# A new order of attention's work on all queues, and the first layer's first two tiles inside the last head

## What is computed

```python
# attention, B, H, S, D = 2, 8, 768, 64
q_bits = (q @ proj > 0); k_bits = (k @ proj > 0)       # 6 bits each -> bucket
mask = q_bucket[..., :, None] == k_bucket[..., None, :]
scores = where(mask, q @ k.T / sqrt(D), -1e9)
scores -= scores.max(-1)
attn = exp(scores); attn /= attn.sum(-1) + 1e-9
x = attn @ v                                           # -> [1536, 512]
# first layer, 512 -> 2048 -> 512
h = maximum(x @ w_in, 0.0); y = h * h @ w_out
# second layer: 8 experts, capacity 192 tokens each, assigned greedily by logit
out[tokens of e] = maximum(y[tokens of e] @ w1[e], 0.0) @ w2[e]
```

## Time and profile before

| | |
|---|---|
| median of 3 runs | 866.53 us (862.17 to 868.55) |
| the profiled execution | 864.65 us, its span 862.9 us, mean granted TensorE clock 0.951 |
| attention | from 0 to about 297 us |
| first layer | to about 582 us |
| routing and experts | to the end |
| busy over the span: DVE, ACT, POOL | 44%, 44%, 46% |

### The profile page before, as it was taken

One profiled execution on the slowest core, in us unless ns is written; L12 is line 12 of the kernel. 1 busy time (PEld: TensorE's weight loads), 2 busy tenths in 40 slices (PEclk: granted clock), 3 DMA queues, 4 the chain that ended last, 5 costly groups with the idle time before them and its releaser, 6 DMA issues. The chain is left out here.

```text
span 862.9 us, 14217 instructions
## 1 busy us (share of the span) xinstructions
PE 787.4 (91%) x4720; PEld 715.8 (83%) x4720; DVE 378.7 (44%) x875; ACT 378.3 (44%) x655; POOL 399.5 (46%) x326
## 2 busy tenths in 40 slices
PE   5999989879996979999999999995399999999986
PEld 3799878768885768999999999984399999899986
DVE  7465656545663245242232224224554455345500
ACT  2676757556674555554554554540012112212221
POOL 5578757565764768655565666560100110111001
PEclk8999999999998989999999999996589999999999
DMA  6465475483845000010000001000343635364531
GB/s 163 101 151 122 108 164 128 102 188 86 192 102 156 1 0 1 0 38 0 0 37 0 0 0 38 0 0 37 131 177 122 230 136 212 118 226 138 192 139 36
DMA packets 43687, 81.38 MB, mean 94 GB/s; under 512 B 17176, under 2 KB 17176, under 8 KB 43136
## 3 DMA queue, kind: packets, MB, share of 16 engines
q1 hardware_dynamic: 41440, 74.58, 30.8%
q0 software_dynamic: 2048, 6.29, 2.2%
q10 hardware_dynamic: 160, 0.00, 0.0%
HBM read 54.55 MB, written 6.29 MB: 71 GB/s over the span
## 5 line engine op out<-in xcount | busy, mean ns | idle before, releaser
L310 POOL TENSOR_TENSOR pt_lo<-pt,pt_hi 128x768 fp32r<-128x768 f32 x64 | 117.7, 1839 | 58.9 <-ACT pt_hi L438 56.5
L1122 PE MATMUL banks<-xt_hi,split_parts 128*128 128x384 f32 (+1 forms) x512 | 141.7, 338 | 0.0
L1133 PE MATMUL banks<-split_parts,h_hi 128*128 128x512 f32 x384 | 122.8, 401 | 5.3 <-DVE h_lo L1048 5.2
L886 POOL TENSOR_TENSOR split_parts<-w_in_sb,split_parts 128x512 fp32r<-128x512 f32 x64 | 84.4, 1319 | 90.3 <-ACT split_parts L879 89.0
L1045 DVE TENSOR_TENSOR h<-relu 128x384 f32<-128x384 f32 x64 | 43.5, 680 | 182.5 <-ACT relu L1000 182.5
L431 ACT ACTIVATE pt<-banks 128x768 f32<-128x768 f32 x96 | 78.0, 813 | 75.5 <-PE banks L683 74.3
L544 DVE TENSOR_REDUCE mx<-banks 128x1 f32<-128x768 f32 x96 | 90.5, 956 | 28.5 <-PE banks L710 24.4
L1566 PE MATMUL banks<-x_cols,w_in_sb 128*128 128x192 f32 x512 | 95.8, 339 | 1.2 <-ACT x_cols L1346 1.1
L1122 PEld LDWEIGHTS banks<-xt_hi,split_parts 128*128 128x128 f32 x512 | 93.7, 188 | 2.9
L1580 PE MATMUL banks<-expert_hidden,w_out_sb 128*128 128x192 f32 x512 | 94.6, 336 | 0.0
L890 POOL TENSOR_TENSOR split_parts<-w_out_sb,split_parts 128x512 fp32r<-128x512 f32 x64 | 84.2, 1315 | 16.2 <-ACT split_parts L882 16.2
(11 more groups left out here) (195 smaller groups left out, 1355.0 us busy)
## 6 DMA issues: line engine op xcount, KB each, us to landing
w_in_sb<-in_moe_w SPq DMA_DIRECT2D x8, 2048.0 KB, 9.8
w_out_sb<-in_moe_w SPq DMA_DIRECT2D x8, 2048.0 KB, 8.6
w_in_sb<-in_moe_w_in SPq DMA_DIRECT2D x8, 512.0 KB, 7.3
w_out_sb<-in_moe_w_out SPq DMA_DIRECT2D x8, 512.0 KB, 5.7
w_out_sb<-in_k SPq DMA_DIRECT2D x16, 192.0 KB, 4.1
w_out_sb<-in_q SPq DMA_DIRECT2D x16, 192.0 KB, 3.4
v_raw<-in_v SPq DMA_DIRECT2D x16, 192.0 KB, 3.8
ka<-split_parts SPq DMA_DIRECT2D x16, 192.0 KB, 4.0
```

The source lines that it names most:

```text
L310: pool.tensor_tensor(pt_lo[x % 2][:], pt[j % 2][:], pt_hi[x % 2][:].bitcast(fp32), ALU.subtract).then_inc(los, 1)
L886: pool.tensor_tensor(wil[i], in_view(f), wih[i].bitcast(fp32), ALU.subtract).then_inc(wils, 1)
L1122: last = pe.matmul(PB[i][:, 0:HALF], w_[:, k, :], x_[:, xs], start=n == 0, stop=n == 3 * DT - 1)
L1133: last = pe.matmul(PB[2 + t][:], h_[:, tc], w_[:], start=start and n == 0, stop=stop and n == 2, skip_group_check=True)
```

## The change

On SyncE the weight transfers go one to each call of `weights` (n from 2 to 13, before: 4 to 12 with two at n = 9 to 11), ka goes ahead of free_row and qb, and the loads of k and q stand behind ka and v. On ScalarE `k_high` stands ahead of the exponential of tile 1, `high(p - 1)` behind that of tile 5, and the first splits of w_in and w_out are in pair 6 and no longer in pair 7. GpSimd follows. TensorE and VectorE have some neighbours exchanged. `hidden` of steps 0 and 1 stands in the last head, with their relu and square between its exponentials; the last head's sums, copy to xt, divisors and low part stand behind the first layer's first steps.

```diff
@@ SyncE
             def weights(n):
-                if 4 <= n < 12:
-                    load_in(sp, n - 4)
-                if 9 <= n < 13:
-                    load_out(sp, n - 9)
+                if 2 <= n < 10:
+                    load_in(sp, n - 2)
+                elif 10 <= n < 14:
+                    load_out(sp, n - 10)
...
             for p in range(PAIRS):
+                asm_kb(2 * p + 1, 1)
+                part_ka(1, p % 2)
                 if p:
                     free_row(2 * p - 1, 1)
-                asm_kb(2 * p + 1, 1)
-                part_ka(1, p % 2)
                 asm_qb(2 * p + 1, 1)
                 if p:
                     load_v(2 * p + 1, 1)
+                weights(2 * p)
                 part_qa(1, p % 2)
+                weights(2 * p + 1)
                 if p + 1 < PAIRS:
                     asm_kb(2 * p + 2, 0)
                     asm_qb(2 * p + 2, 0)
                     free_row(2 * p, 0)
+                    part_ka(0, (p + 1) % 2)
+                    load_v(2 * p + 2, 0)
+                more_k(p + 3)
                 more_q(p + 3)
-                weights(2 * p)
-                if p + 1 < PAIRS:
-                    load_v(2 * p + 2, 0)
-                    part_ka(0, (p + 1) % 2)
-                more_k(p + 3)
-                weights(2 * p + 1)
                 if p + 1 < PAIRS:
                     part_qa(0, (p + 1) % 2)
@@ GpSimd
             for p in range(PAIRS):
-                if p:
-                    low(p - 1)
+                if p + 2 < PAIRS:
+                    k_low(pool, p + 2)
                 low_part(2 * p, 1)
...
                 v_low_part(2 * p + 1, 1)
                 if p + 2 < PAIRS:
                     q_low(pool, p + 2)
-                    k_low(pool, p + 2)
+                if p + 2 == PAIRS:
+                    split["in_low"](pool, 0, 0, 0)
+                    split["in_low"](pool, 1, 1, 1)
+                    split["out_low"](pool, 0, 0, 0)
+                if p:
+                    low(p - 1)
                 low_part(2 * p + 1, 1)
...
-                if p + 1 == PAIRS:
-                    split["in_low"](pool, 0, 0, 0)
-                    split["in_low"](pool, 1, 1, 1)
-                    split["out_low"](pool, 0, 0, 0)
                 divide(p, 0)
                 divide(p, 1)
...
-            low(PAIRS - 1)
+            later["low"] = lambda: low(PAIRS - 1)
@@ ScalarE
             for p in range(PAIRS):
                 expo(2 * p, 0)
-                high(p - 1)
                 sums(2 * p - 1, 1)
+                k_high(p + 2)
+                if p + 2 == PAIRS:
+
+                    for taken in (ka_in, kb_in, qa_in, qb_in):
+                        act.wait_ge(taken[0], 32 * (PAIRS - 1) - (16 if taken in (kb_in, qb_in) else 0))
+                        act.wait_ge(taken[1], 32 * (PAIRS - 1))
+                    act.wait_ge(split["w_early"], 16 * 9)
+                    split["in_high"](act, 0, 0)
+                    split["in_high"](act, 1, 1)
+                    split["out_high"](act, 0, 0)
                 expo(2 * p, 1)
                 expo_high(2 * p, 1)
-                k_high(p + 2)
...
                 expo(2 * p, 4)
-                if p + 1 == PAIRS:
...
+                v_high(2 * p + 1, 1)
                 expo_high(2 * p, 4)
                 expo(2 * p, 5)
+                high(p - 1)
+                row(2 * p + 1, 1)
                 q_high(p + 2)
-                row(2 * p + 1, 1)
                 v_sum_high(2 * p + 1)
-                v_high(2 * p + 1, 1)
...
                 expo(2 * p + 1, 4)
+                if p + 1 == PAIRS:
+                    split["tile"](act, 0, 0)
                 expo_high(2 * p + 1, 4)
                 expo(2 * p + 1, 5)
-                v_sum_high(2 * p + 2)
                 row(2 * p + 2, 0)
                 v_high(2 * p + 2, 0)
-            sums(HEADS - 1, 1)
-            high(PAIRS - 1)
+                v_sum_high(2 * p + 2)
+            split["tile"](act, 1, 1)
+            later["sums"] = lambda: sums(HEADS - 1, 1)
+            later["high"] = lambda: high(PAIRS - 1)
@@ VectorE
+                    q_bits(p + 1, qbit[w]).then_inc(qbits, 1)
                     k_bits(p + 1, kbit[w]).then_inc(kbits, 1)
-                    q_bits(p + 1, qbit[w]).then_inc(qbits, 1)
...
+                sum_v(2 * p + 1, 1)
                 row_max(2 * p + 1, 5)
-                sum_v(2 * p + 1, 1)
...
-            turn(HEADS - 1, 1, 0)
-            turn(HEADS - 1, 1, 1)
-            reciprocals(HIGH)
-            dve.drain()
+            def last_divisors(h):
+                turn(HEADS - 1, 1, h)
+                if h:
+                    reciprocals(HIGH)
@@ TensorE
+            def early_hidden(g):
+
+                if g == 0:
+                    pe.wait_ge(mxs, 6 * HEADS - 1)
+                    pe.wait_ge(xl, 5)
+                split["hidden"](pe, g, 0, g)
+
             def pair(p, w, first, last):
 
-                if not last:
-                    z_k(p + 1, w)
+                if not first:
+                    weigh(2 * p - 1, 1, 5)
                 scores_t(2 * p, 0, p, 0)
                 if not first:
-                    weigh_low(2 * p - 1, 1, 4)
-                    weigh(2 * p - 1, 1, 5, False, True)
-                scores_t(2 * p, 0, p, 1)
+                    weigh_low(2 * p - 1, 1, 4, False, True)
                 if not last:
                     z_q(p + 1, w)
+                    z_k(p + 1, w)
+                scores_t(2 * p, 0, p, 1)
                 weigh(2 * p, 0, 0, True)
...
                 weigh(2 * p, 0, 5)
+                weigh_low(2 * p, 0, 4)
                 scores_t(2 * p + 1, 1, p, 0)
-                weigh_low(2 * p, 0, 4)
                 weigh_high(2 * p, 0, 4, False, True)
...
                 scores_t(2 * p + 1, 1, p, 2)
+                if last:
+                    early_hidden(0)
...
+                fallback(2 * p + 1, 1, 0)
+                scores_t(2 * p + 1, 1, p, 4)
+                if last:
+                    early_hidden(1)
                 weigh_low(2 * p + 1, 1, 1)
-                scores_t(2 * p + 1, 1, p, 4)
-                fallback(2 * p + 1, 1, 0)
-                weigh_high(2 * p + 1, 1, 3)
                 weigh_low(2 * p + 1, 1, 2)
                 fallback(2 * p + 1, 1, 1)
+                weigh_high(2 * p + 1, 1, 3)
@@ weight_splits: hidden and tile, used by both stages
+    def tile(act, g, i):
+        act.wait_ge(hid, g + 1)
+        act.activation(r32[i][:], PB[i][:, 0:HALF], ACT.Relu).then_inc(relus, 1)
+        act.wait_ge(relus, g + 1)
+        act.activation(hh[i][:], r32[i][:], ACT.Square).then_inc(hhs, 1)
@@ first layer, GpSimd
             for g in range(6):
                 both_low(g, g + 2, g + 1, g % 2)
+                if g == 1:
+                    later["low"]()
@@ first layer, ScalarE
-                tile_high(c * FT, 2, 1, 0, None if first else c - 1)
-                tile_high(c * FT + 1, 3, 2, 1)
                 if first:
+
+                    in_high(2, 2, 0)
+                    out_high(1, 1, 1)
+                    later["sums"]()
+                    in_high(3, 3, 1)
+                    out_high(2, 2, 0)
+                    later["high"]()
                     for g in range(2, 8):
                         tile_high(g, g + 2, g + 1, g % 2)
@@ first layer, VectorE
                     if first:
-                        if j == 1:
+                        if j < 2:
+                            later["divisors"](j)
+                        elif j == 3:
@@ first layer, TensorE
-            hidden(0, 0, 0)
             chunk(0, 0, HALF, True, False)
```

More of the change, by code:

```diff
@@ L93, in attention @@
         more_bits = sb("more_bits", [P, S])
+        later = {}
         kbit = (spare[:, SPARE + 2 * S:SPARE + 3 * S], spare[:, SPARE - S:SPARE])
@@ L615, in pair @@
                     row_max(2 * p + 2, 5)
+                    sum_v(2 * p + 2, 0)
                     max_done(2 * p + 2)
-                    sum_v(2 * p + 2, 0)
                 invert(p)
@@ L639, in _ @@
             pair(PAIRS - 1, 0, False, True)
-            turn(HEADS - 1, 1, 0)
-            turn(HEADS - 1, 1, 1)
-            reciprocals(HIGH)
-            dve.drain()
+            def last_divisors(h):
+                turn(HEADS - 1, 1, h)
+                if h:
+                    reciprocals(HIGH)
+            later["divisors"] = last_divisors
         @block.tensor
@@ L837, in _ @@
             pair(PAIRS - 1, 0, False, True)
-            weigh_low(HEADS - 1, 1, 4)
-            weigh(HEADS - 1, 1, 5, False, True)
+            weigh(HEADS - 1, 1, 5)
+            weigh_low(HEADS - 1, 1, 4, False, True)
+        return later
 def routing_constants(nc, ctx):
@@ L870, in weight_splits, with hidden @@
     wihs, wils, wohs, wols = (sem("split_" + n) for n in ("wihs", "wils", "wohs", "wols"))
+    hid, relus, hhs = (sem("first_" + n) for n in ("hid", "relus", "hhs"))
```

(50 more changed lines are left out.)

41 lines of the change are left out of this document (17 added, 24 removed).

## The result

| | before | changed kernel |
|---|---|---|
| median | 865.95 us (862.17 to 868.55, 4 runs) | 837.34 us (835.10 to 841.54, 4 runs) |
| ratio | | 0.9679, 95% interval 0.9626 to 0.9731 |
| profiled execution | 864.65 us, span 862.9 | 841.54 us, span 839.8 |

The forecast was 837 (828 to 849).

What follows compares the result with a forecast made beforehand. TensorE, busy 91% of the span, was taken as the bound, so only its stalls could be won: 36.3 us removed less 6.7 back, net 29.6, from the 866.53 us median to 837 us (828 to 849).

Steps and rivals of the forecast that it cites:

- Part 1: Order of the loads on SyncE: TensorE's waits for qa in pairs 3 to 6 go, 19.2 us removed.
- Part 2: Copy to xt_hi behind the head's scores: the last pair's first half loses 9.5 us, with 0.4 us back.
- The wait that I named next: Last pair: first weigh waits for VectorE's two transposes with only four matmuls as cover, 0.4 us back.
- Part 3: k_high ahead of the exponential of tile 1 on ScalarE: fits between sums and tile 1's scores, priced at 0.
- Part 4: First weight splits moved to pair 6: ScalarE waits for qa, TensorE idles 4.6 us; cost 6.3 us, bounds 2 and 9.
- Part 5: Two first-layer tiles inside the last head: h_lo wait and half-clock rows(0) go, 7.1 us, plus 0.5 for pt_lo.
- rival C: Entry of the first layer keeps a wait, 3 to 5 us with half clock: 841 us, chance 0.10.
- the sign of being wrong on part 5: Entry of the first layer: h_lo or the low part of w_in is waited for.
- A: Pair 6's wait does not appear, as ScalarE's wait ends within TensorE's cover: 831 us, chance 0.16.
- D: Nothing is won, since the stalls come back elsewhere in the cycle: 858 to 866 us, chance 0.07.
- B: The load queue stays late and half of the 19.2 us remains: 847 us, chance 0.14.
- E: Pairs 0 to 5: ScalarE's wait for ka ahead of tile 1's exponential stalls TensorE; 871 us at 9 us landing, chance 0.03.

Runs made afterwards that it cites:

- The old order: The kernel with the late splits, with TensorE's and VectorE's order within a pair as before the change: 826.92 us, and 828.37 us when run again.
- the kernel with a gap of 3.85: The changed kernel with pair 6's two weight transfers behind all its other loads: 833.71 us.
- the late splits: The changed kernel with the first weight splits later, ScalarE's behind the odd head's row copy in pair 6, GpSimd's at pair 7's start: 829.48 and 828.47 us.

## Why the prediction was right

**Part 1** (19.2 us forecast). Right in mechanism and size: 18.5 us in pairs 1 to 5, 19.5 with the loads alone. The sum of bytes behind asm_kb against 247 GB/s was enough to see that qa would be in time. In pair 2 of the changed kernel its last half is issued at 107.20 us and lands 4.6 us later, 29.5 us into the pair, where I had 27 and TensorE wants it at 33.

**Part 2** (9.5 less 0.4). 8.6 us measured. The wait that I named next is there, but for the exponential of tile 1 and not for the transposes: 0.55 us at 251.63 in the changed kernel, with scores_t of that tile now right behind weigh_low. The old order shows the wait for the transposes instead, 0.6 us. Either way half a microsecond.

**Part 3** (0). Right. ScalarE shows no wait ahead of its copy of k in any pair of the changed kernel: in pair 1 it starts at 57.29 us, as the sums end.

**Part 4** (6.3 back, bounds 2 and 9). Right in mechanism, undersized: 10.1 us (26.85 less the 16.72 of a first half without a stall), just past my upper bound. Two terms were short. The landing: I took it at 235.0 us, 10.8 after the pair's start at 224.16, and it came 13.7 after (219.46 less 205.72), 2.9 late, by the two weight transfers beside qa and by scatter. And the half clock: I took 1.7 us from pairs 3 and 5. Here it was 2.7 (10.13 less 7.43) and, in the kernel with a gap of 3.85, 2.7 too (its first half took 23.24). Pairs 4 and 7 had shown more before: 5.59 of excess for 3.52 of idle, 9.53 for 6.79. I had these rows and took the cheaper ones.

**Part 5** (7.6 with the wait for pt_lo). 7.67 us: the size is right, and the wait for h_lo is gone as forecast. But I wrote the gain up as the tiles covered by their place, and that is 1.0 of it. The rest lies in what stood ahead of relu, GpSimd's three splits, the division, the sums and the copy. I had named that chain as the cause of the wait, but gave the splits' leaving it to part 4, as a cost alone; which link is worth how much stays open. A wait of 0.50 us for w_in's low part, behind GpSimd's divisions, is what I had as rival C, at a tenth to a sixth of its price; I had also set a wait for that low part as the sign of being wrong on part 5, and by it the part is not clean. VectorE's h steps in the last head were shorter than feared: 0.56 and 0.56 us for the first tile (GpSimd had nothing then), 0.56 and 1.49 for the second; the earlier trace rows had 1.75 for one beside GpSimd.

```profile
276.43 0.56 DVE L1089 TENSOR_TENSOR h<-relu 128x384 f32<-128x384 f32 x1 [7.30 <-ACT relu L908]
277.06 0.56 DVE L1092 TENSOR_TENSOR h_lo<-h,h_hi 128x384 fp32r<-128x384 f32 x1
...
283.79 1.49 DVE L1092 TENSOR_TENSOR h_lo<-h,h_hi 128x384 fp32r<-128x384 f32 x1
```

**The sum.** In the profiled executions I forecast -29.6 us. Up to the end of the first layer it was -26.3, 3.3 short, nearly all of it part 4; the second layer added 3.2 that have nothing to do with the change, -23.1 in all. The medians differ by 28.6. That 837 was met to 0.3 us is in part luck, then: part 4 cost 4 us more than I said in its profile, and the median ran lower than the profile by as much. Of the rivals, A and D did not happen, B and E left no trace, C happened at 0.5 us.

## What to carry to other kernels

Where an engine is full between its stalls, cut its time at a repeated event and price each stretch against the cleanest one: what an order can win is the excess. More than half of it was had here by moving transfers alone (19.5 of the 36 us that the late splits win up to there). A wait in an in-order queue costs by what stands behind it; here one block of 1.7 us of work, put one position too early behind a transfer, cost 10 us of TensorE, six times itself, and moved half a pair later it was free. When a large edit wins, take its parts singly: the loads, the copy, and what no longer stands ahead of the first relu carry nearly all of it, and the exchanged neighbours on TensorE and VectorE nothing. And take them apart to the end: what was won at the end of attention, 6.7 us of it, is left with two possible causes, because the move that looked like a pure cost (the weight splits, out of pair 7) may also be what freed GpSimd at the end of attention.

## What the runs showed of the hardware that was not expected

- The same code scatters in its transfers' landing: 6.9, 6.4 and 4.9 us for pair 6's qa (192 KB) in three profiles of the same code up to there, with a transfer of 512 KB ahead of it and one behind. Without them it took 3.8 and 4.3 us in two.
- The second layer, the same tensor work in all kernels here, took from 274.2 to 281.8 us from the first layer's last matmul on h_hi to the end, over 14 profiles. Single profiles of two kernels can differ by 7 us with no cause in the change. In the two profiles at the ends of this range TensorE's weight loads waited 3.3 and 6.8 us for the gathered rows, which is half of the difference; the other half stays open.
- What the half clock adds does not follow the length of the gap. In the profiles of pair 6 it added 2.7, 3.1, 2.5, 2.4, 3.0 and 2.7 us after gaps of 3.85, 4.01, 5.50, 6.47, 6.96 and 7.43 us; in the earlier trace rows 1.7 us for 3.68 and for 5.75 us of idle, and 2.1 for 3.52. In the changed kernel the granted clock was 0.50 from 222.0 to 227.0 us and 1.00 from 228.0; in pair 3 of the kernel before 0.50 from 120.0 to 122.0 and 1.00 from 123.0.
